# Expert tokens in one tile of 384 each and then in blocks of 128, in a fused attention, MLP and mixture-of-experts kernel

## The chip, the core and the metric

The kernel runs on one core of one Trainium2 chip. The metric is the device time of a run in microseconds (us). The engines are named as the profile names them: PE is TensorE (PEld its weight loads), DVE is VectorE, ACT is ScalarE, POOL is GpSimd, SP is the queue that issues most DMAs.

## The reference

```
N, D, E, F = 2304, 512, 8, 1024
x = attention(q, k, v)                  # 4 x 8 heads, 576 positions, window 128
x = (s * relu(x @ w_in)**2 + b) @ w_out # 512 -> 2048 -> 512
logits = x @ w_gate
noisy  = logits + log1p(exp(x @ w_noise)) * noise
top2, top2_w = the two largest of 8, softmax of the two
for e in range(8):
    for k in range(2):
        mask = top2[:, k] == e
        h = max(x[mask] @ w1[e], 0)
        out[mask] += top2_w[mask, k] * (h @ w2[e])
```

Each of the 2304 tokens goes to two of the eight experts, so the experts see 4608 token rows. With the inputs of the reference (a fixed seed) its own routing, worked out from its formulas, gives the experts 514, 463, 581, 704, 662, 654, 542 and 488 tokens.

## The kernel before, in words

All matrix products take a value as a rounded part and a rest (`..._hi` and `..._lo`) and make three matmuls of it (`three`, L1132 to L1134).

Stage one (T1 = 6 tiles of 384 tokens) interleaves the attention with the dense MLP; in each tile a loop over 16 chunks of the hidden size makes a slot of 12 matmuls over 384 columns (`first_product`) and 9 over 512 (`second_product`). The routing of the tile before is threaded through the slots: `turn_x2` transposes its output, `logits` (L1158) multiplies it with `w_route` so that the logits come out as 16 rows, DVE copies them (`copy_logits`, L788) and `turn_logits` (L1165) transposes them; `choose` and `assign` then find experts and places, and POOL scatters each token row (512 values and 4 words that go with it: two weights, its place, its number) to two rows of `rows_scratch` in DRAM. `rows_scratch` and `y_scratch` are partly filled with zeros by SP in the first tile's slots (L404, L407).

Stage two is the experts. A short table (DVE, `table`) holds how many tiles of TOK2 = 256 tokens an expert has, at least two; the last tile of an expert is moved back so that it ends with its last token, and tiles may so overlap. A loop runs over the tiles of an expert on each engine, with the engines held together by semaphores that count tiles. One tile `i`:

- SP: `load_rows(i + 1)` (L417) after the rows before are turned and after DVE has read the words that go with them (`meta_used`); in the first tile of an expert it also loads the next expert's eight weight chunks; after `r_ready` it writes the result to `y_scratch` (L436).
- PE: eight chunks `c`, `first_product` with 128 rows of weights as the stationary operand and the 256 tokens as the moving one (12 matmuls of 256 columns) and, two chunks later (`LAG`), `second_product` with the hidden values stationary and 512 weight columns moving (6 matmuls of 512 columns); `turn_rows(i + 1)` (L1257, eight transposes) stands two `second_product`s from the end.
- ACT: relu into `g_hi` (L679), the next expert's weights (L667), then the rounding of the turned rows (L661).
- DVE: the rest `g_lo` (L1024), `indices` and `whole_indices` (the index words, L983 to L1007), the rests of the weights (L1015) and of the rows (L959), and last the result `x2` (L1039), weight times product plus what was fetched.
- POOL: gathers the other expert's share of each token from `y_scratch` (L493) and scatters the result to the output (L501). A token's second expert adds the first one's result to its own.

The buffers are single: `rows`, `xm_hi`, `xm_lo` hold one tile, so the load of the next rows waits until the words that go with the rows of this one are read.

Of the kernel before, what the change touches and what calls it, by code (L numbers as in the profile page):

```python
# [9 lines left out]
ALU = mybir.AluOpType  # L10
# [3 lines left out]
P = 128  # L14
# [19 lines left out]
TOK2, BLK2 = 256, 2  # L34
NBLK = N // P
GMAX = N * 2 // TOK2 + 2 * E
# [65 lines left out]
def build(nc, a, out):  # L102
# [8 lines left out]
    with ctx:  # L111
# [12 lines left out]
        logits_t = sb("logits_t", [2 * E, TOK1], F32)  # L124
# [41 lines left out]
        out_to = sb("out_to", [P, BLK2], I32)  # L166
        first_row = sb("first_row", [P, E + 1], F32)
# [92 lines left out]
        lg_copied = sem("lg_copied")  # L260
        lg_turned = sem("lg_turned")
# [22 lines left out]
        tile_done = sem("tile_done")  # L284
# [5 lines left out]
        out_done = sem("out_done")  # L290

# [44 lines left out]
        def tile_at(eng, e, least_at):  # L336

            return eng.value_load(bounds[0:1, bass.ds(e, 1)], min_val=least_at, max_val=GMAX - 2 + least_at)

        def tiles_of(eng, pr, par):  # L340

            return tile_at(eng, pr * 2 + par, 0), tile_at(eng, pr * 2 + par + 1, 2)

        with nc.Block() as block:
            @block.sync
            def _(sp):
# [48 lines left out]
                for t in range(T1):  # L395
                    for c in range(C1 + LAG):
# [18 lines left out]
                def load_rows(i):  # L415
                    r = 0 if isinstance(i, int) else sp.value_load(starts[0:1, bass.ds(i, 1)], min_val=0, max_val=ROWS - TOK2)
                    sp.dma_start(rows[:], rows_dram[bass.ds(r, TOK2), :].rearrange("(b p) d -> p b d", p=P)  # L417
                                 ).then_inc(rows_in, 16)

                def tile(i, chunks=None):  # L420
                    if chunks is not None:
                        q0, ks = chunks
                        for k in ks[:C2 // 2]:
                            load_weights(sp, load_later(sp, q0 + k), k % STAGES)
                    sp.wait_ge(turned, i * BLK2 + BLK2)
# [4 lines left out]
                    if chunks is not None:  # L430
                        for k in ks[C2 // 2:]:
                            load_weights(sp, load_later(sp, q0 + k), k % STAGES)
# [15 lines left out]
                with sp.Fori(0, E // 2 - 1) as pr:  # L448
                    for par in range(2):
                        expert(pr, par, range(STAGES, STAGES + C2))  # L450
# [897 lines left out]
```

## Time and profile before

| | |
|---|---|
| time, median of three runs | 1155.73 us (1154.34 to 1157.4) |
| time of the profiled execution | 1154.33 us |
| its span, first to last instruction | 1152.5 us |
| mean granted TensorE clock | 0.973 |
| PE busy | 1076.9 us, 93% |
| DVE busy | 677.6 us, 59% |
| ACT busy | 476.9 us, 41% |
| POOL busy | 137.3 us, 12% |

The profile is one execution. A busy PE means only that matmuls were in flight, so the pace of the matmuls (start to start) is read from the timeline and from the chain of waits. The chain is followed back from the last instruction, at each step to what released it. The granted clock is given as a share of full speed: 1.00 is 2.4 GHz, 0.50 is 1.2 GHz, and what lies between is a mean over a stretch.

### The profile page before, as it was taken

How to read it: one execution, taken by the hardware profiler on the slowest of the kernel's cores; microseconds unless marked ns; L12 is line 12 of the kernel's file. 1: busy time of each engine (PE TensorE's matmuls, PEld its weight loads, DVE VectorE, ACT ScalarE, POOL GpSimd, SP SyncE). 2: the span in 40 equal slices, each digit the busy share in tenths (PEclk: the TensorE clock that was granted, in tenths of full speed). 3: DMA queues.
4: the chain of work that ended last, by engine and by line, in shares of the span. 5: the costliest groups of instructions: out<-in, count | busy, mean ns of one | idle time of the engine just before them, and what ended most of it. 6: DMA issues, size and time to landing. Idle time of an engine off the chain costs nothing.

```text
span 1152.5 us, 20528 instructions
## 1 busy us (share of the span) xinstructions
PE 1076.9 (93%) x6751; PEld 965.5 (84%) x6752; DVE 677.6 (59%) x2006; ACT 476.9 (41%) x1036; POOL 137.3 (12%) x135
## 2 busy tenths in 40 slices
PE   5699799999999999999974999999999999999995
PEld 4588698888888888888854999999999999999994
DVE  6777566866866776754756537463635537354342
ACT  6656465555555555534532314231413214132111
POOL 0000000100110020020012211212121212112121
PEclk9799999999999999999996999999999999999998
DMA  6559922342342242132353515161522516243232
GB/s 186 148 193 361 324 79 87 105 126 92 101 134 90 84 161 74 44 109 88 121 172 108 168 37 185 63 208 49 183 83 90 192 61 206 95 137 104 69 107 73
DMA packets 80238, 146.90 MB, mean 127 GB/s; under 512 B 12924, under 2 KB 13564, under 8 KB 80176
## 3 DMA queue, kind: packets, MB, share of 16 engines
q1 hardware_dynamic: 70256, 125.36, 33.9%
q0 software_dynamic: 9920, 20.78, 5.3%
q8 instruction: 30, 0.49, 0.2%
q14 instruction: 32, 0.26, 0.1%
HBM read 111.14 MB, written 46.77 MB: 137 GB/s over the span
## 4 chain that ended last, share of the span: by engine, by line
PE 81%; DVE 5%; ACT 5%; issue 4%; SPq 3%; DMA 1%; POOL 0%; POOLq 0%; DVEq 0%; ACTq 0%
PE bank L1132 24%; PE bank L1133 23%; PE bank L1134 23%; PE bank L1113 3%; PE bank L1257 2%; PE bank L1100 2%; PE bank L1158 1%; ACT x_sc L525 1%; PE bank L1079 1%; SPq L351 1%; PE bank L1080 1%; DVE x_sc L721 1%; ACT w_now_hi L579 1%; SPq L407 1%; ACT qk_hi L513 1%
## 5 line engine op out<-in xcount | busy, mean ns | idle before, releaser
L679 ACT ACTIVATE g_hi<-bank 128x256 fp32r<-128x256 f32 x176 | 67.7, 384 | 347.7 <-PE bank L1134 331.6
L1024 DVE SCALAR_TENSOR_TENSOR g_lo<-bank,g_hi 128x256 fp32r<-128x256 f32 x176 | 74.5, 423 | 183.3 <-ACT g_hi L679 183.2
L1132 PE MATMUL bank<-w_hi,g_hi 128*128 128x512 f32 x336 | 136.0, 405 | 0.0
L1133 PE MATMUL bank<-w_lo,g_hi 128*128 128x512 f32 x336 | 131.8, 392 | 0.0
L1134 PE MATMUL bank<-w_hi,g_lo 128*128 128x512 f32 x336 | 131.2, 391 | 0.0
L585 ACT ACTIVATE relu<-bank 128x384 f32<-128x384 f32 x96 | 47.1, 490 | 168.4 <-PE bank L1134 159.3
L1132 PE MATMUL bank<-xm_hi,w_hi 128*128 128x256 f32 x384 | 109.1, 284 | 1.5 <-DVE xm_lo L959 1.5
L1134 PE MATMUL bank<-xm_hi,w_lo 128*128 128x256 f32 x384 | 109.3, 285 | 0.0
L1133 PE MATMUL bank<-xm_lo,w_hi 128*128 128x256 f32 x384 | 109.3, 285 | 0.0
L468 POOL DMA_INDIRECT rows_scratch<-x,slot x36 | 38.4, 1067 | 533.0 <-DVE x L861 523.9
L776 DVE SCALAR_TENSOR_TENSOR relu<-relu,sb_scale 128x384 f32<-128x384 f32 x96 | 59.3, 618 | 65.8 <-ACT relu L585 64.6
L1134 PE MATMUL bank<-xm_hi,w_other_lo 128*128 128x256 f32 x320 | 90.6, 283 | 0.0
L1133 PE MATMUL bank<-xm_lo,w_other_hi 128*128 128x256 f32 x320 | 90.5, 283 | 0.0
L1132 PE MATMUL bank<-xm_hi,w_other_hi 128*128 128x256 f32 x320 | 90.2, 282 | 0.0
L1132 PEld LDWEIGHTS bank<-xm_hi,w_hi 128*128 128x128 f32 x384 | 74.2, 193 | 4.9 <-issue 1.9
L525 ACT ACTIVATE x_sc<-x_sc,least 128x256 f32<-128x256 f32 (+1 forms) x144 | 69.9, 488 | 19.0 <-DVE least L721 18.7
L1133 PEld LDWEIGHTS bank<-xm_lo,w_hi 128*128 128x128 f32 x384 | 74.2, 193 | 2.8
L493 POOL DMA_INDIRECT spare<-y_scratch,y_from x44 | 51.4, 1169 | 202.6 <-DVEq L1009 171.7
L1134 PEld LDWEIGHTS bank<-w_hi,g_lo 128*128 128x128 f32 x336 | 63.1, 188 | 14.2
L770 DVE TENSOR_TENSOR w_now_lo<-stage_a,w_now_hi 128x1024 fp32r<-128x1024 f32 x48 | 58.6, 1221 | 27.8 <-ACT w_now_hi L579 25.1
L1134 PEld LDWEIGHTS bank<-xm_hi,w_lo 128*128 128x128 f32 x384 | 74.1, 193 | 0.0
L721 DVE CUSTOM_DVE_ANT_0 x_sc<-bank,nbias 128x256 f32<-128x256 f32 (+1 forms) x144 | 52.9, 405 | 34.5 <-PE bank L1080 26.3
(177 smaller groups left out, 2774.8 us busy)
## 6 DMA issues: line engine op xcount, KB each, us to landing
stage_a<-in_w_first SPq DMA_DIRECT2D x92, 256.0 KB
stage_a<-in_w_second SPq DMA_DIRECT2D x92, 256.0 KB
y_scratch<-x SPq DMA_DIRECT2D x41, 512.0 KB, 7.2
qk_raw<-in_qk SPq DMA_DIRECT2D x144, 128.0 KB, 2.7
rows<-rows_scratch SPq DMA_DIRECT2D x23, 516.0 KB
stage_b<-in_w_first SPq DMA_DIRECT2D x28, 256.0 KB
stage_b<-in_w_second SPq DMA_DIRECT2D x28, 256.0 KB
v_sb<-in_vp SPq DMA_DIRECT2D x18, 256.0 KB, 2.9
```

The lines of the kernel that those rows point to most:

```text
L468: pool.indirect_dma_start(out=rows_dram, out_offset=bass.IndirectOffsetOnAxis(ap=slot[:, j, k:k + 1], axis=0), in_=x2[:, j, :], in_offset= ...
L493: pool.indirect_dma_start(out=fetched[:, j, :], out_offset=None, in_=y_dram, in_offset=bass.IndirectOffsetOnAxis(ap=y_from[:, j:j + 1], ax ...
L525: done = act.activation(x_sc[:, i % XS, s, 0:keys], x_sc[:, i % XS, s, 0:keys], ACT.Exp, scale=-1.0, bias=least[:, hp, s:s + 1], accum_out ...
L585: act.activation(relu[:, (t * C1 + c) % GR, :], h_bank[c % 2][:, 0:TOK1], ACT.Relu).then_inc(relu_ready, 1)
L679: act.activation(g_hi[:, c % GR, 0:TOK2], h_bank[c % 2][:, 0:TOK2], ACT.Relu).then_inc(gh2_ready, 1)
L721: done = dve.tensor_tensor_reduce(out=x_sc[:, i % XS, s, 0:keys], in0=s_of(i)[:, s * 256:s * 256 + keys], in1=nbias[:, 2 * hp + s, first:f ...
L770: dve.tensor_tensor(ring_a(1, p), stage(r % EARLY), ring_a(0, p).bitcast(F32), ALU.subtract).then_inc(w_ready, 1)
L776: dve.scalar_tensor_tensor(out=r, in0=r, scalar=sb_scale[:, 0:1], in1=r, op0=ALU.mult, op1=ALU.mult).then_inc(sq_ready, 1)
L1024: dve.scalar_tensor_tensor(out=g_lo[:, c % GR, 0:TOK2], in0=h_bank[c % 2][:, 0:TOK2], scalar=0.0, in1=g_hi[:, c % GR, 0:TOK2].bitcast(F32) ...
L1132: pe.matmul(psum, lh, rh, start=(first and n == 0), stop=False)
L1133: pe.matmul(psum, lh, rl, start=False, stop=False)
L1134: done = pe.matmul(psum, ll, rh, start=False, stop=(last and n == len(pairs) - 1))
```

## The change

Each expert now takes one tile of 384 tokens (`tile(e)`, TOK2 = 384), built as before but with three blocks of 128, and then blocks of 128 tokens (`single`), at least one. With the counts above that is 8 tiles and 2, 1, 2, 3, 3, 3, 2 and 1 blocks, 17 in all. The weights of the next expert are loaded and split in the tile.

In a block both products have 128 tokens as the stationary operand and 512 weight columns as the moving one: `block_first` makes the 1024 hidden values in two halves (12 matmuls each), with tokens down the partitions; relu goes to `hidden`, `turn_hidden` transposes a half (four transposes), ACT rounds it to `gb_hi` and DVE makes `gb_lo`; `block_second` makes eight chunks of three matmuls. `turn_block(i + 1)`, four transposes of the next block's rows, stands half way through the `block_second`s. The block has its own semaphores (`b_...`) and its own row buffer `rows_1`, also single. On DVE the increment of `b_meta_used`, for which SP waits before `load_block(i + 1)`, stands behind both halves of `gb_lo`. On POOL a block has one gather and one scatter.

In stage one the logits are made with the tokens stationary and `w_route` moving (16 columns), so they come out by tokens: `copy_logits` and `turn_logits` are gone, and `logits` moves from slot 3 to slot 5. `fetched` and the table's work space lie in `x2T`. The zero writes are 24 of 258 KB and 13 of 768 KB (before: 16 of 258 KB and 19 of 512 KB), and `y_scratch` is zeroed up to slot 14 in place of slot 11.

The core of the diff (left out: semaphores, POOL's part, the table's formulas, the parts of `tile` that only change names):

```diff
-TOK2, BLK2 = 256, 2
+TOK2, BLK2 = 384, 3
 NBLK = N // P
-GMAX = N * 2 // TOK2 + 2 * E
+GMAX = (2 * N - 2 * TOK2) // P + E
...
-        logits_t = sb("logits_t", [2 * E, TOK1], F32)
...
+        xb_hi = sb("xb_hi", [P, KD, P], F32R)
+        xb_lo = sb("xb_lo", [P, KD, P], F32R)
         rows = sb("rows", [P, BLK2, RW], F32)
-        spare = sb("spare", [P, 4 * G * E], F32)
+        rows_1 = sb("rows_1", [P, 1, RW], F32)
+        spare = x2T[:].rearrange("p k n -> p (k n)")
...
+        hidden = relu[:].rearrange("p r n -> p (r n)")[:, 0:F2]
+        gb_hi = g_hi[:].rearrange("p r n -> p (r n)")[:, 0:F2]
+        gb_lo = g_lo[:].rearrange("p r n -> p (r n)")[:, 0:F2]
...
+        b_out, b_rows, b_turned = bank[0], bank[2], bank[6:8]
...
-                            for r in range((c - 2) * 2 * TOK2, min((c - 1) * 2 * TOK2, YROWS), TOK2):
-                                sp.dma_start(y_dram[r:r + TOK2, :].rearrange("(p b) d -> p b d", b=2),
-                                             x2[:, 1:3, 0:DM]).then_inc(zero_out, 16)
+                            for r in range((c - 2) * TOK2, min((c - 1) * TOK2, YROWS), TOK2):
+                                sp.dma_start(y_dram[r:r + TOK2, :].rearrange("(p b) d -> p b d", b=BLK2),
+                                             x2[:, :, 0:DM]).then_inc(zero_out, 16)
...
+                def load_block(i):
+                    r = sp.value_load(starts[0:1, bass.ds(i, 1)], min_val=0, max_val=ROWS - P)
+                    sp.dma_start(rows_1[:], rows_dram[bass.ds(r, P), :].rearrange("(b p) d -> p b d", p=P)
+                                 ).then_inc(b_rows_in, 16)
...
+                def tile(e, later, ks):
+                    for k in ks[:C2 // 2]:
+                        load_weights(sp, load_later(sp, e * C2 + k), k % STAGES)
+                    if later:
+                        sp.wait_ge(turned, e * BLK2 + BLK2)
+                        sp.nop(nofuse=True)
+                        sp.wait_ge(meta_used, e + 1)
+                        sp.nop(nofuse=True)
+                        load_rows(e + 1)
+                    for k in ks[C2 // 2:]:
+                        load_weights(sp, load_later(sp, e * C2 + k), k % STAGES)
+                    sp.wait_ge(r_ready, e + 1)
                     sp.nop(nofuse=True)
-                    sp.wait_ge(meta_used, i + 1)
+                    r = sp.value_load(y_first[0:1, bass.ds(e, 1)], min_val=0, max_val=YROWS - TOK2)
+                    sp.dma_start(y_dram[bass.ds(r, TOK2), :].rearrange("(b p) d -> p b d", p=P),
+                                 x2[:, :, 0:DM]).then_inc(y_out, 16)
+
+                def single(i):
+                    sp.wait_ge(b_turned_x, i + 1)
                     sp.nop(nofuse=True)
-                    load_rows(i + 1)
-                    if chunks is not None:
-                        for k in ks[C2 // 2:]:
-                            load_weights(sp, load_later(sp, q0 + k), k % STAGES)
-                    sp.wait_ge(r_ready, i + 1)
+                    sp.wait_ge(b_meta_used, i + 1)
+                    sp.nop(nofuse=True)
+                    load_block(i + 1)
+                    sp.wait_ge(b_r_ready, i + 1)
                     sp.nop(nofuse=True)
                     r = sp.value_load(y_starts[0:1, bass.ds(i, 1)], min_val=0, max_val=YROWS - TOK2)
-                    sp.dma_start(y_dram[bass.ds(r, TOK2), :].rearrange("(b p) d -> p b d", p=P),
-                                 x2[:, 0:BLK2, 0:DM]).then_inc(y_out, 16)
-
-                def expert(pr, par, ks):
-                    lo, hi = tiles_of(sp, pr, par)
-                    tile(lo, ((pr * 2 + par) * C2, ks) if ks else None)
-                    with sp.Fori(lo + 1, hi) as i:
-                        tile(i)
+                    sp.dma_start(y_dram[bass.ds(r, P), :].rearrange("(b p) d -> p b d", p=P),
+                                 x2[:, 0:1, 0:DM]).then_inc(b_y_out, 16)
+
+                def expert(e, later, ks):
+                    tile(e, later, ks)
+                    with sp.Fori(first_of(sp, e), end_of(sp, e)) as i:
+                        single(i)
...
+                def single(i):
+                    for half in range(2):
+                        cols = slice(half * DM, (half + 1) * DM)
+                        act.wait_ge(b_h_ready, i * 2 + half + 1)
+                        act.activation(hidden[:, cols], h_bank[half][:], ACT.Relu).then_inc(b_relu_ready, 1)
+                        act.wait_ge(b_h_turned, i * 2 + half + 1)
+                        act.activation(gb_hi[:, cols], b_turned[half][:], ACT.Copy).then_inc(b_gh_ready, 1)
+                    round_block(i + 1)
+
+                def expert(e, par, more=True, later=True):
+                    lo = first_of(act, e)
+                    tile(e, lo, more, (1 - par) * C2, later)
+                    with act.Fori(lo, end_of(act, e)) as i:
+                        single(i)
...
+                def rest_of_block(i):
+                    dve.wait_ge(b_xh_ready, i + 1)
+                    dve.tensor_tensor(xb_lo[:], b_rows[:].rearrange("p (k n) -> p k n", k=KD),
+                                      xb_hi[:].bitcast(F32), ALU.subtract).then_inc(b_xl_ready, 1)
...
+                            dve.wait_ge(rows_in, e * 16 + 16)
+                            indices(meta, e, rows[:, :, DM:RW], BLK2, region[:, 0, bass.ds(e, 1)], y_from[:])
+                            dve.sem_inc(meta_ready, 1)
                         if c == 4:
-                            whole_indices(i)
-                        if q0 is not None:
-                            rest_of_later(q0, c, other + c)
-                    rest_of_rows(i + 1)
-                    dve.wait_ge(tile_done, i + 1)
-                    dve.wait_ge(fetched_in, i * (BLK2 * 16) + BLK2 * 16)
-                    dve.wait_ge(y_out, i * 16)
-                    dve.wait_ge(out_done, i * (BLK2 * 16))
+                            dve.wait_ge(out_done, e * (BLK2 * 16))
+                            dve.tensor_scalar(out_to[:], sought[:, 1, :], NOWHERE, None, ALU.add
+                                              ).then_inc(meta_used, 1)
...
+                def single(e, i):
+                    dve.wait_ge(b_rows_in, i * 16 + 16)
+                    indices(b_meta, i, rows_1[:, :, DM:RW], 1, start_f[:, bass.ds(i, 1)], y_from_1[:])
+                    dve.sem_inc(b_meta_ready, 1)
+                    for half in range(2):
+                        cols = slice(half * DM, (half + 1) * DM)
+                        dve.wait_ge(b_gh_ready, i * 2 + half + 1)
+                        dve.tensor_tensor(gb_lo[:, cols], b_turned[half][:], gb_hi[:, cols].bitcast(F32), ALU.subtract
+                                          ).then_inc(b_gl_ready, 1)
+                    dve.wait_ge(b_out_done, i * 16)
+                    dve.tensor_scalar(out_to_1[:], sought[:, 1, 0:1], NOWHERE, None, ALU.add).then_inc(b_meta_used, 1)
+                    rest_of_block(i + 1)
+                    dve.wait_ge(b_done, i + 1)
+                    dve.wait_ge(b_fetched_in, i * 16 + 16)
+                    dve.wait_ge(y_out, e * 16 + 16)
+                    dve.wait_ge(out_done, e * (BLK2 * 16) + BLK2 * 16)
+                    dve.wait_ge(b_y_out, i * 16)
+                    dve.scalar_tensor_tensor(out=x2[:, 0, 0:DM], in0=b_out[:], scalar=w_tile[:, 0:1],
+                                             in1=fetched[:, 0, :], op0=ALU.mult, op1=ALU.add).then_inc(b_r_ready, 1)
...
-                            done = pe.matmul(to[0:2 * E, j * P:(j + 1) * P], w_route[:, k, :],
-                                             x2T[:, k, j * P:(j + 1) * P], start=(k == 0), stop=(k == KD - 1))
+                            done = pe.matmul(to[:, j * 2 * E:(j + 1) * 2 * E], x2T[:, k, j * P:(j + 1) * P],
+                                             w_route[:, k, :], start=(k == 0), stop=(k == KD - 1))
...
+                def turn_block(i):
+                    pe.wait_ge(b_rows_in, i * 16 + 16)
+                    for k in range(KD):
+                        done = pe.transpose(b_rows[:, k * P:(k + 1) * P], rows_1[:, 0, k * P:(k + 1) * P], ident[:])
+                    done.then_inc(b_turned_x, 1)
...
+                def block_first(par, half, ks):
+                    w = (w_hi, w_lo) if par == 0 else w_other
+                    cs = slice(half * C2 // 2, (half + 1) * C2 // 2)
+                    for k in ks:
+                        done = three(h_bank[half][:], [
+                            (xb_hi[:, k, :], xb_lo[:, k, :], w[0][:, cs, k * P:(k + 1) * P],
+                             w[1][:, cs, k * P:(k + 1) * P])], k == 0, k == KD - 1)
+                    return done
+
+                def turn_hidden(i, half):
+                    pe.wait_ge(b_relu_ready, i * 2 + half + 1)
+                    for k in range(KD):
+                        at_ = half * DM + k * P
+                        done = pe.transpose(b_turned[half][:, k * P:(k + 1) * P], hidden[:, at_:at_ + P], ident[:])
+                    done.then_inc(b_h_turned, 1)
+
+                def block_second(par, cs):
+                    w = (w_hi, w_lo) if par == 0 else w_other
+                    for c in cs:
+                        done = three(b_out[:], [
+                            (gb_hi[:, c * P:(c + 1) * P], gb_lo[:, c * P:(c + 1) * P],
+                             w[0][:, c, DM:CW], w[1][:, c, DM:CW])], c == 0, c == C2 - 1)
+                    return done
+
+                def single(e, par, i, later):
+                    pe.wait_ge(b_xl_ready, i + 1)
+                    block_first(par, 0, range(KD)).then_inc(b_h_ready, 1)
+                    block_first(par, 1, range(KD // 2))
+                    if later:
+                        pe.wait_ge(xl2_ready, e + 2)
+                    turn_hidden(i, 0)
+                    block_first(par, 1, range(KD // 2, KD)).then_inc(b_h_ready, 1)
+                    pe.wait_ge(r_ready, e + 1)
+                    pe.wait_ge(b_r_ready, i)
+                    pe.wait_ge(b_gl_ready, i * 2 + 1)
+                    block_second(par, range(C2 // 4))
+                    turn_hidden(i, 1)
+                    block_second(par, range(C2 // 4, C2 // 2))
+                    turn_block(i + 1)
+                    pe.wait_ge(b_gl_ready, i * 2 + 2)
+                    block_second(par, range(C2 // 2, C2)).then_inc(b_done, 1)
+
+                def expert(e, par, later=True):
+                    lo = first_of(pe, e)
+                    tile(e, par, lo, later)
+                    with pe.Fori(lo, end_of(pe, e)) as i:
+                        single(e, par, i, later)
```

## Rows read from the trace of the kernel before

**Rows 1.** Stretches: us, each engine's busy us (instructions), clock, DMA share, GB/s.
```profile
623.14:1140.05 516.91, 516.89 (x3344) 470.83 (x3344) 254.71 (x692) 144.66 (x276) 94.04 (x86) 1.00 0.36 118
...
160.00:590.00 430.00, 423.71 (x2608) 376.82 (x2607) 292.30 (x890) 231.03 (x521) 32.34 (x30) 1.00 0.33 104
...
84.00:130.00 46.00, 44.07 (x269) 39.36 (x268) 34.10 (x87) 29.27 (x65) 0.00 (x0) 1.00 1.04 354
```

**Rows 2.** Chain of waits in stage two: start us, us, engine and line.
```profile
632.04 0.23 PE bank L1132
...
634.86 0.23 PE bank L1132
...
668.16 0.87 PE bank L1257 x8
...
691.57 0.87 PE bank L1257 x8
```

**Rows 3.** Groups by form: operation, count, busy us, mean ns, idle time before.
```profile
L1132 PE MATMUL bank<-xm_hi,w_hi 128*128 128x256 f32 x384 | 109.1, 284 | 1.5 <-DVE xm_lo L959 1.5
...
L1132 PE MATMUL bank<-xm_hi,w_other_hi 128*128 128x256 f32 x320 | 90.2, 282 | 0.0
...
L1039 DVE SCALAR_TENSOR_TENSOR x<-bank,w_tile,spare 128x512 f32<-128x512 f32 x44 | 31.0, 746 | 31.2 <-PE bank L1134 31.2
...
L959 DVE TENSOR_TENSOR xm_lo<-bank,xm_hi 128x512 fp32r<-128x512 f32 x46 | 29.7, 685 | 28.6 <-ACT xm_hi L661 28.6
L661 ACT ACTIVATE xm_hi<-bank 128x512 fp32r<-128x512 f32 x46 | 25.1, 596 | 43.0 <-PE bank L1257 43.0
...
L1007 DVE TENSOR_SCALAR out_to<-sought 128x2 int32<-128x2 f32 x22 | 3.5, 159 | 0.0
```

**Rows 4.** Timeline of PE in stage one: start us, us, the matmul.
```profile
562.02 0.33 PE L1132 MATMUL bank<-x_hi,w_hi 128*128 128x384 f32 x1
...
564.13 0.39 PE L1132 MATMUL bank<-w_hi,g_hi 128*128 128x512 f32 x1
```

**Rows 5.** Timelines of ACT, DVE and SP around a transpose and a load.
```profile
692.04 1.09 ACT L661 ACTIVATE xm_hi<-bank 128x512 fp32r<-128x512 f32 x2 [1.36 <-PE bank L1257]
...
655.17 0.23 DVE L997 TENSOR_TENSOR sought<-sought,role 128x2 f32<-128x2 f32 x2
...
656.33 0.40 SPq L417 DMA_DIRECT2D rows<-rows_scratch  x1
```

**Rows 6.** The page, part 6: DMA, count, KB each, median us to landing.
```profile
y_scratch<-x SPq DMA_DIRECT2D x41, 512.0 KB, 7.2
...
v_sb<-in_vp SPq DMA_DIRECT2D x18, 256.0 KB, 2.9
```

**Rows 7.** Chain of waits, the first load of rows.
```profile
615.86 3.71 DMA rows<-rows_scratch
```

**Rows 8.** Stretches around idle gaps of PE; columns as in rows 1.
```profile
41.80:44.20 2.40, 0.17 (x2) 0.00 (x0) 1.47 (x4) 1.85 (x5) 0.29 (x1) 1.00 0.57 162
...
46.40:50.90 4.50, 0.35 (x2) 0.00 (x0) 3.15 (x10) 2.52 (x6) 0.00 (x0) 0.50 0.56 160
...
134.50:139.39 4.89, 0.24 (x2) 0.03 (x1) 3.55 (x11) 3.61 (x9) 0.00 (x0) 0.91 1.06 392
139.39:143.10 3.71, 3.71 (x33) 3.38 (x33) 2.35 (x5) 1.37 (x2) 0.00 (x0) 0.50 0.59 168
...
145.00:148.00 3.00, 3.00 (x18) 2.83 (x17) 0.60 (x4) 1.09 (x3) 0.00 (x0) 0.95 0.02 5
...
66.70:70.10 3.40, 3.40 (x15) 3.30 (x14) 3.06 (x9) 2.62 (x7) 0.00 (x0) 0.51 0.67 222
```

**Rows 9.** Chain of waits between the two stages, the last logits.
```profile
595.89 2.81 PE bank L1158 x24
...
598.72 0.56 DVE logits_t L788
...
599.32 0.37 PE bank L1165 x3
```

More of the change, by code:

```diff
@@ L483, in _, with tile @@
                     scatter(t)
-                pool.wait_ge(table_ready, 1)
-                n_tiles = pool.value_load(bounds[0:1, E:E + 1], min_val=1, max_val=GMAX)
-                with pool.Fori(0, n_tiles) as i:
-                    pool.wait_ge(meta_ready, i + 1)
-                    pool.wait_ge(y_out, i * 16)
+                def tile(e):
+                    pool.wait_ge(meta_ready, e + 1)
+                    pool.wait_ge(y_out, e * 16)
+                    pool.wait_ge(b_y_out, first_of(pool, e) * 16)
                     pool.nop(nofuse=True)
@@ L667, in round_later, with tile @@
                     act.activation(ring(0, place), stage(k % STAGES), ACT.Copy).then_inc(w_hi_done, 1)
-                def tile(i, q0=None, other=0, after=None):
-                    hi = None
+                def tile(e, lo, more, other, later):
                     for c in range(C2):
-                        if after is not None and c == C2 - 2:
-                            hi = tile_at(act, after, 2)
-                        act.wait_ge(h2_ready, i * C2 + c + 1)
+                        act.wait_ge(h2_ready, e * C2 + c + 1)
@@ L683, in tile @@
-                    round_rows(i + 1)
-                    return hi
-                def expert(pr, par, lo, more=True):
-                    hi = tile(lo, (pr * 2 + par) * C2 if more else None, (1 - par) * C2, pr * 2 + par + 1)
-                    with act.Fori(lo + 1, hi) as i:
-                        tile(i)
-                    return hi
+                            act.wait_ge(b_done, lo)
+                        act.activation(g_hi[:, c % GR, :], h_bank[c % 2][:, 0:TOK2], ACT.Relu).then_inc(gh2_ready, 1)
@@ new lines, in tile @@
+                        if more:
+                            round_later(e * C2, c, other + c)
+                    if later:
+                        round_rows(e + 1)
+                def single(i):
[6 more added lines that the diff above has]
+                    round_block(i + 1)
@@ L998, in indices @@
                     link(done)
[L999 to L1007 removed]
+                    dve.memset(fetched[:, 0:nb], 0.0)
@@ L1016, in rest_of_later, with tile @@
                                       ).then_inc(w_ready, 1)
-                def tile(i, q0=None, other=0, after=None):
-                    hi = None
+                def tile(e, lo, more, other, later):
                     for c in range(C2):
-                        if after is not None and c == C2 - 2:
-                            hi = tile_at(dve, after, 2)
-                        dve.wait_ge(gh2_ready, i * C2 + c + 1)
-                        dve.scalar_tensor_tensor(out=g_lo[:, c % GR, 0:TOK2], in0=h_bank[c % 2][:, 0:TOK2],
-                                                 scalar=0.0, in1=g_hi[:, c % GR, 0:TOK2].bitcast(F32),
+                        dve.wait_ge(gh2_ready, e * C2 + c + 1)
+                        dve.scalar_tensor_tensor(out=g_lo[:, c % GR, :], in0=h_bank[c % 2][:, 0:TOK2],
+                                                 scalar=0.0, in1=g_hi[:, c % GR, :].bitcast(F32),
@@ L1038, in tile @@
+                        if more:
+                            rest_of_later(e * C2, c, other + c)
+                    if later:
+                        rest_of_rows(e + 1)
+                    dve.wait_ge(chunk2_used, e * C2 + C2)
+                    dve.wait_ge(fetched_in, e * (BLK2 * 16) + BLK2 * 16)
+                    dve.wait_ge(y_out, e * 16)
+                    dve.wait_ge(b_y_out, lo * 16)
+                    dve.wait_ge(b_out_done, lo * 16)
                     for j in range(BLK2):
@@ L1041, in tile, with single @@
                     done.then_inc(r_ready, 1)
-                    return hi
-                def expert(pr, par, lo, more=True):
-                    hi = tile(lo, (pr * 2 + par) * C2 if more else None, (1 - par) * C2, pr * 2 + par + 1)
-                    with dve.Fori(lo + 1, hi) as i:
-                        tile(i)
-                    return hi
+                def single(e, i):
+                    dve.wait_ge(b_rows_in, i * 16 + 16)
[16 more added lines that the diff above has]
+                                             in1=fetched[:, 0, :], op0=ALU.mult, op1=ALU.add).then_inc(b_r_ready, 1)
@@ L1050, in _, with expert @@
+                def expert(e, par, more=True, later=True):
+                    lo = first_of(dve, e)
+                    tile(e, lo, more, (1 - par) * C2, later)
+                    with dve.Fori(lo, end_of(dve, e)) as i:
+                        single(e, i)
                 rest_of_rows(0)
+                rest_of_block(0)
                 with dve.Fori(0, E // 2 - 1) as pr:
-                    lo = tile_at(dve, pr * 2, 0)
                     for par in range(2):
-                        lo = expert(pr, par, lo)
```

251 lines of the change are left out of this document (126 added, 125 removed).

## The prediction

> **What bounds the kernel now.** I read first the busy time of each engine by stretch. The reader is to see that PE is the bound of both stages: 516.89 of 516.91 us in stage two, with the clock at 1.00 throughout, and 423.71 of 430 us in five sixths of stage one [rows 1]. No other engine is near that. Then I read the chain of waits in stage two, which is PE from end to end. The reader is to see two periods: 2.82 us from chunk to chunk (632.04 to 634.86) and 23.41 us from tile to tile (668.16 to 691.57), with the eight transposes of the next rows at 0.87 us in it, 0.109 each [rows 2]. A chunk is 12 matmuls of 256 columns and 6 of 512; at 0.23 for one of 512 [rows 2] that leaves 0.12 for one of 256. The groups by form give the tiles: 384 and 320 matmuls of one kind, 32 to a tile, are 12 and 10 tiles [rows 3], as the routed counts say (3, 2, 3, 3, 3, 3, 3, 2). So stage two is worth what PE's work in it is worth, as long as nothing stops PE. Last I looked for places where PE did stop, since the change gives it new waits; these are in the stretches around gaps [rows 8].
>
> **PE's work in stage two.** Before: 22 tiles of 256 are 5632 token slots. After: 8 x 384 + 17 x 128 = 5248. A slot of a 384 tile is 12 matmuls of 384 columns, which took 2.11 us in stage one (562.02 to 564.13) [rows 4], and 9 of 512 at 0.232 (between the 0.23 and 0.24 at which they run), 2.09; eight slots are 33.6. Eight tiles with seven times 12 transposes at 0.109 are 278.0. A block is 48 matmuls of 512 columns, 11.14, and 12 transposes, 1.31, together 12.45; 17 are 211.6. With 1.6 for the half clock at the start, as now, that is 491.2 against 516.9: minus 25.7. Without the 120 more transposes (13 us) it would be minus 39.
>
> **The wait that a block adds.** In `single` PE goes: half 0 (12 matmuls), two more of half 1's four steps, `turn_hidden(0)`, the rest of half 1, two chunks of `block_second`, `turn_hidden(1)`, two chunks, `turn_block(i + 1)`, four chunks. `turn_block(i + 1)` waits for `rows_1`; SP issues that load only after `b_meta_used`, and this increment stands on DVE behind both halves of `gb_lo`. So the load starts late, and I count from the start of `turn_hidden(1)`: 0.47 until ACT starts (691.57 to 692.04) [rows 2, 5]; the rounding 0.60 and the rest 0.69 [rows 3], with 0.06 between; the index operation 0.16 [rows 3]; 0.93 from the end of such a DVE operation (655.40) to SP's issue (656.33), in which SP reads the row number [rows 5]; the landing of 258 KB; 0.14 to PE. A load of 256 KB lands in 2.9 [rows 6], the load of two blocks of rows (516 KB) in 3.71 [rows 7]; I take 2.95, as the size is nearly that of the first. Sum 6.0 us. In that time PE has `turn_hidden(1)`, 0.44, and 6 matmuls, 1.40. PE then stands for 4.2 us, in each of the 17 blocks: plus 71.1. Bounds: 0.8 more each with the other landing, plus 14; nothing in the order of DVE's or SP's instructions lets it be less than about 3. Queued behind PE's wait are 12 matmuls, the next block or tile, and so all of ACT's and DVE's work.
>
> On the fixed part of that landing, the Trainium skill (DMA: Bandwidth & Descriptors, Anatomy of one DMA) has about 2.0 us for any DMA of POOL's path plus the bytes at 436 GB/s; by that, as an estimate, 258 KB take 2.6 us and the sum would be 5 us less. The load here goes by SP's queue, and the row of 2.9 decides.
>
> In an expert's first block a write of 768 KB to `y_scratch` comes just ahead of the load, on the same queue; writes of 512 KB took 7.2 [rows 6]. Issued 3.4 us after the tile's end (three result operations at 0.75 [rows 3], 0.93 of SP) it would still be landing when the load is issued at 10.5 (7.44 of PE's work in the block, then 3.05 of the chain above). I take 0.6 more for each of eight, plus 5 (0 to 10). The same write also delays the gather of the first block to some 16 us; the block ends at 16.7 and its result is needed 6 us later: nothing.
>
> The other waits of a block, worked out with the same durations: relu of half 0 is ready 0.6 us before PE wants it; `gb_lo` of half 0 ends as PE wants it (5.99 against 6.04); DVE's result operation and indices are over by then; `turn_block` to the next block's rests takes 1.8 us under 2.8 us of matmuls. Nothing, at most 0.2 a block. In a tile DVE has 33.6 us for the work it did in 23, and the next expert's weights land earlier against their use: nothing.
>
> **The clock.** An idle gap of 4.2 us has two like it in this trace. In the stretch of 46.40 to 50.90 PE was busy for 0.35 us and the clock at 0.50 all through; in that of 134.50 to 139.39 it was busy for 0.24, idle for 4.65, and the clock fell some 0.9 us before the end (0.91 over 4.89 us). A shorter one, 2.2 us idle in 41.80 to 44.20, kept 1.00 [rows 8]. After the fall PE ran at 0.50 from 139.39 until about 145.3, 5.9 us; another cold stretch lasted 3.4 us (66.70 to 70.10) [rows 8]. At half clock half the stretch is lost: 2.95 or 1.7, mean 2.3. As the fall came only just inside the gap of 4.65, I let seven in ten of the 17 gaps end cold: 17 x 0.7 x 2.3 = 27.6. Bounds: 0, and 17 x 3.2 = 54.7, if all that follows the gap in a block (four transposes and 12 matmuls) runs at half.
>
> **Stage one and the joints.** The logits keep 24 matmuls a tile (2.81 us [rows 9]), with 16 columns moving in place of 128 but 128 columns of weights in place of 16. From above they cost as the transposes do, which load as many (0.109, 2.6 us); from below I have only that the moving part shrinks, and let it go to 1.6. I take 2.1. With the three small transposes that is 1.0 a tile, minus 5 for five tiles (1 to 8), in a stage where PE is the bound. On the way to stage two the copy (0.56), the transposes (0.37) [rows 9] and 0.7 of logits fall away; a third block of rows brings 0.8 of landing (the 3.71 against 2.9 above) and 0.75 of rounding and rest: minus 0.1. At the end one of two result operations falls away (0.75 [rows 3]): minus 0.7; the one scatter less is left at nil.
>
> The zero writes grow from 13.9 to 16.2 MB. To slot 9 they come at the old rate, in a stretch where the DMA engines are full (share 1.04, 354 GB/s [rows 1]) and PE nonetheless busy; 2.3 MB more, 6.5 us at that rate, fall into slots 11 to 14, where PE's gap before 139.39 stands. I take plus 2 (minus 3 to plus 6.5).
>
> **Sum.** 1152.5 - 25.7 + 71.1 + 5 + 27.6 - 5 - 0.1 - 0.7 + 2 = 1226.7 of span; 1.8 lie around it (1154.33 - 1152.5), so 1228.5 for such an execution, whose time before was 1.4 below the median of the runs. I predict 1228.
>
> **The rivals.**
> - The clock holds in the gaps, as in that of 2.2 us: minus 27.6, 1201. For it: the fall at 4.65 came late in the gap. Against it: both gaps over 4 us ended at half.
> - The clock falls in each gap and the rest of the block is cold: plus 27, 1255. The Trainium skill (TensorE: Matmul & The Clock Gate, HAM oscillation) has this for a loop that waits for a DMA in each pass: it falls to the half rate in each. By that rule it would be 1255; the two long gaps here agree with it.
> - The load takes longer, beside gather, scatter and write of the same blocks: 1.5 us more in 17 blocks is 25, 1254. For it: writes of twice the size took 7.2 [rows 6].
> - Other side, faster: the rows of the next block are there when PE comes for them, so that neither stall, contention nor clock cost anything: 1228.5 - 71.1 - 5 - 27.6 = 1125. It decides at 1.7 us a block: 29.5 us are gained without stalls, over 17. For it is only that DMAs land in 3 us while a block lasts 12.5; against it is that the load's issue is tied to the last third of the block.
> - The change doesn't do what it says, as the counts of blocks differ: each block more or less is 18 us with its stall. The 12 and 10 tiles speak for the counts.
>
> **How the numbers follow.** Forecast, with its own range of 1210 to 1246: 0.45. Clock falls each time: 0.2. Clock holds: 0.15. Longer load: 0.1. Hidden load: 0.05. The rest, 0.05, lies outside on both sides. The range of 1192 to 1258 takes in the first four. A measurement can tell about 0.3% (3.5 us) from no change: faster 0.05, same 0.02, slower 0.93.
>
> **What would show it.** In the changed profile: the group of `turn_block`'s transposes with 17 or 18 waits on the DMA of `rows_1`, some 4 us each; before it SP waiting for DVE; a granted clock under 1.00 in the stretches of blocks and 1.00 in the tiles; a tile in 34.9 us and a block in 16.7 warm, 19 cold; more bytes written at 130 to 145 us. I am wrong if the load is issued before `turn_hidden(1)`, if it lands in under 1 us, or if another wait in a block (the second rest, the fetched rows) is longer than this one.

## The result and the profile after

The changed kernel takes 1234.17 us, median of 6 runs (1228.59 to 1235.94), beside 1155.45 us (1152.99 to 1157.58) of the kernel before: a ratio of 1.068, 95% interval 1.066 to 1.070. The forecast was 1228, range 1192 to 1258. The profiled execution has a span of 1226.8 us; the sum of the forecast gave 1226.7. That execution, at 1228.59 us, is the fastest of the six. Measured once more, beside the later experiments, the changed kernel was at 1.065 (1.063 to 1.068).

First the stretches of the changed kernel: stage two, the tail, and then one block (677.32 to 695.57) cut at its wait. Columns are us, busy us of PE, PEld, DVE, ACT and POOL with instructions, granted clock, DMA share, GB/s.

```profile
623.45:1216.97 593.52, 528.77 (x2448) 449.08 (x2448) 240.78 (x658) 146.39 (x226) 83.91 (x81) 0.93 0.30 98
1216.97:1226.80 9.83, 0.17 (x1) 0.00 (x0) 0.75 (x1) 0.00 (x0) 1.01 (x1) 0.64 0.14 53
...
677.32:686.82 9.50, 9.39 (x45) 7.28 (x43) 4.06 (x19) 2.39 (x4) 2.05 (x2) 1.00 0.08 29
686.99:690.74 3.75, 0.00 (x1) 0.01 (x1) 0.02 (x1) 0.00 (x0) 0.00 (x0) 0.99 0.28 70
690.74:694.17 3.43, 3.43 (x11) 2.90 (x11) 0.69 (x1) 0.60 (x1) 0.00 (x0) 0.51 0.02 5
694.17:695.57 1.40, 1.40 (x8) 1.13 (x6) 0.00 (x0) 0.00 (x0) 0.00 (x0) 1.00 0.00 0
```

Stage two lasts 593.5 us where it lasted 516.9 [rows 1], 76.6 more, which is the whole loss (the span grew by 74.3, as the tail is shorter); it begins at 623.45 where it began at 623.14. PE is no longer busy throughout (528.77 of 593.52), and the clock is at 0.93. In the block all engines are idle for 3.75 us while 16 DMA engines are 28% busy, and after it PE runs at half clock for 3.4 us.

The waits of PE in stage two (what waited, for whom, us in total, times, longest):

```profile
PE bank L1327 <- DMA rows<-rows_scratch: 62.9, 17, 3.9
```

L1327 is the transposes of `turn_block`. Before, PE waited 16.3 us in all for such a load, once, ahead of the stage; now 17 times more, once in each block. The only other wait in the list for this stage is one of 0.8 us; waits as short as 0.1 us are not in it. The chain of waits through one of the 17 (start us, us, what):

```profile
685.15 0.45 PE bank L1362 x4
...
685.63 0.61 ACT g_hi L751
...
686.26 0.05 DVE g_lo L1108
686.31 0.55 issue
686.87 0.16 DVE out_to L1111
...
687.10 0.05 SPq L442
...
687.92 2.77 DMA rows<-rows_scratch
...
690.74 1.12 PE bank L1327 x4
```

This is the path that was counted out beforehand: the turn of the second half (L1362), the rounding, the rest (the "issue" of 0.55 is the body of that operation), the index operation, SP's reading of the row number (L442), the load and the transposes. From the turn's start at 684.99 to 690.74 it is 5.75 us, where the forecast had 6.0. The landing took 2.77 for 2.95 and the step from DVE to SP's issue 0.90 for 0.93; the start of the rounding came 0.64 us behind the turn's start for 0.47.

### The profile page after: what moved, and what is told of

Read it like the earlier page. It is cut to its first block, busy times and chain, and to the rows that moved or that the text cites. A ratio compares the mean times of both kernels' runs of the same rounds, so it can differ in the third digit from the quotient of the medians.

```text
span 1226.8 us, 18393 instructions
## 1 busy us (share of the span) xinstructions
PE 1088.4 (89%) x5845; PEld 948.0 (77%) x5846; DVE 661.0 (54%) x1967; ACT 480.1 (39%) x988; POOL 126.5 (10%) x130
## 4 chain that ended last, share of the span: by engine, by line
PE 76%; issue 6%; DMA 5%; DVE 5%; ACT 5%; SPq 1%; POOL 0%; ACTq 0%; DVEq 0%; POOLq 0%
PE bank L1208 22%; PE bank L1209 21%; PE bank L1210 21%; DMA rows<-rows_scratch 4%; PE bank L1189 3%; PE bank L1176 2%; PE bank L1327 1%; PE bank L1234 1%; PE bank L1155 1%; ACT x_sc L583 1%; PE bank L1362 1%; PE bank L1320 1%; PE bank L1156 1%; DMA stage_a<-in_w_second 1%; ACT g_hi L751 1%
## 5 line engine op out<-in xcount | busy, mean ns | idle before, releaser
L739 ACT ACTIVATE g_hi<-bank 128x384 fp32r<-128x384 f32 x64 | 31.5, 492 | 170.9 <-PE bank L1210 168.1
L1076 DVE SCALAR_TENSOR_TENSOR g_lo<-bank,g_hi 128x384 fp32r<-128x384 f32 x64 | 35.6, 556 | 82.9 <-ACT g_hi L739 76.0
L1327 PE MATMUL bank<-ident,rows 128*128 128x128 f32 x72 | 19.1, 418 | 62.9 <-DMA rows<-rows_scratch 62.9
L1208 PEld LDWEIGHTS bank<-w_hi,g_hi 128*128 128x128 f32 x312 | 62.9, 201 | 15.3 <-issue 4.6
L1208 PE MATMUL bank<-w_other_hi,g_hi 128*128 128x512 f32 x160 | 71.2, 445 | 0.9
L1209 PEld LDWEIGHTS bank<-w_lo,g_hi 128*128 128x128 f32 x312 | 62.7, 201 | 10.1
L1208 PE MATMUL bank<-x_hi,w_hi 128*128 128x384 f32 x192 | 67.3, 351 | 1.8 <-DVE x_lo L809 1.7
L749 ACT ACTIVATE relu<-bank 128x512 f32<-128x512 f32 x34 | 20.3, 598 | 123.4 <-PE bank L1210 123.4
L1209 PE MATMUL bank<-w_other_lo,g_hi 128*128 128x512 f32 x160 | 68.6, 429 | 0.0
L1210 PE MATMUL bank<-w_other_hi,g_lo 128*128 128x512 f32 x160 | 68.1, 426 | 0.0
L1208 PE MATMUL bank<-x_hi,w_now_hi 128*128 128x384 f32 x192 | 66.8, 348 | 0.1
L1327 PEld LDWEIGHTS bank<-ident,rows 128*128 128x128 f32 x72 | 12.5, 210 | 70.2 <-DMA rows<-rows_scratch 70.2
```

The lines of the kernel that those rows point to most:

```text
L1076: dve.scalar_tensor_tensor(out=g_lo[:, c % GR, :], in0=h_bank[c % 2][:, 0:TOK2], scalar=0.0, in1=g_hi[:, c % GR, :].bitcast(F32), op0=ALU. ...
L1208: pe.matmul(psum, lh, rh, start=(first and n == 0), stop=False)
L1209: pe.matmul(psum, lh, rl, start=False, stop=False)
L1210: done = pe.matmul(psum, ll, rh, start=False, stop=(last and n == len(pairs) - 1))
L1327: done = pe.transpose(b_rows[:, k * P:(k + 1) * P], rows_1[:, 0, k * P:(k + 1) * P], ident[:])
```

## The experiments

The kernels were measured in two groups, each on one chip together with the kernel before. It gave 1151.58 us beside the early leave, the fills of 16 and 8 matmuls and the logits alone, and 1153.84 beside the others; ratios are to it, and times of different groups are compared by ratio.

### The leave given early

The increment for which SP waits moves up; the one left behind goes to a new semaphore for which nothing waits.

```diff
                     dve.sem_inc(b_meta_ready, 1)
+                    dve.sem_inc(b_meta_used, 1)
...
-   dve.tensor_scalar(out_to_1[:], sought[:, 1, 0:1], NOWHERE, None, ALU.add).then_inc(b_meta_used, 1)
+   dve.tensor_scalar(out_to_1[:], sought[:, 1, 0:1], NOWHERE, None, ALU.add).then_inc(b_out_to, 1)
```

> The kernel after the change, with one edit: in a block DVE gives SP leave to load the next block's rows right behind the index words, in place of behind both rests of the hidden values. Theory (the late leave makes the wait, 3.9 us in each of 17 blocks, and the clock that falls in that gap costs 2.1 more in each): both go, 66 + 36 us, and the time is 1132 us (1128 to 1142), the clock 1.00 through the blocks. Rival (a block of 128 tokens has a second wait just behind the first, the relu, turn and rounding chain or the gather of what is added): the wait moves, PE still stands over 2 us a block and the time stays over 1165.

Measured: 1132.6 us (1129.66 to 1134.97), ratio 0.983 (0.981 to 0.986). Its stage two, and PE's waits in it:

```profile
624.59:1122.28 497.69, 493.55 (x2448) 424.11 (x2448) 240.77 (x658) 146.46 (x227) 83.89 (x81) 1.00 0.36 117
```

```profile
PE bank L1329 <- DMA rows<-rows_scratch: 2.0, 4, 1.0
PE bank L1210 <- DVE xm_lo L1022: 0.6, 1, 0.6
PE bank L1210 <- DVE g_lo L1110: 0.2, 1, 0.2
```

Moving one semaphore increment takes 95.8 us out of stage two (593.5 to 497.7). The wait for the rows falls from 62.9 us to 2.0 and no wait takes its place that is longer than it was (the short one for the first rest, 0.28 us a block, was there before and is still), so the rival, a second wait close behind, falls. The changed kernel with this edit beats both kernels, the one before by 1.7%.

### The gap filled with matmuls

```diff
                     block_second(par, range(C2 // 4, C2 // 2))
+                    w_any = w_hi if par == 0 else w_other[0]
+                    for _ in range(16):
+                        pe.matmul(bank[1][:], gb_hi[:, 0:P], w_any[:, 0, DM:CW], start=True, stop=True)
                     turn_block(i + 1)
```

> The kernel after the change, with 16 more matmuls of 512 columns in each block ahead of the transposes that wait for the rows, into a bank that nobody reads (results are unchanged). They take 3.7 us, the length of the idle gap, so the load is as late as before but PE isn't idle. Theory (66 us of the loss are the wait and 36 the half clock after it): only the clock's part goes, 1234 - 36 = 1198 us, clock 1.00. Rival (the clock costs nothing of its own, as the chain of the next block has slack for it): 1234, unchanged.

Measured: 1193.84 us (1188.77 to 1194.69), ratio 1.037 (1.035 to 1.039). Stage two:

```profile
620.22:1177.16 556.94, 554.74 (x2720) 472.75 (x2720) 240.67 (x658) 146.51 (x226) 84.09 (x81) 1.00 0.32 105
```

PE has 272 more matmuls to do and the kernel is faster than the changed one, at a ratio of 1.037 for 1.065, which is 32 us. The load is as late as before: a block takes as long up to `turn_block`. All that differs is that PE isn't idle, and the clock stays at 1.00. In the profiles stage two is 593.5 - 556.9 = 36.6 us shorter. The transposes began 0.1 us sooner in each block, 1.7 us of it, so the clock by itself costs 35 us. That fits what the changed profile has: 16 stretches from `turn_block` to the end of a block took 33.4 us more than the 3.25 that each takes here, and the last one, cut short by the end of the stage, 1.6 more. From 556.9 to 497.7, 59.2 us, is the wait by itself.

With 8 of these matmuls:

> As the one with 16 added matmuls, but with 8 (1.9 us), which leave PE idle for about 2.0 us in each block. Theory (a short gap leaves the clock alone, as one of 2.2 us did before the change): 1198 us, as with 16. Rival (any gap of 2 us in each block is enough): half clock after the gaps and 1215 to 1234.

Measured: 1192.53 us (two executions, 1191.11 and 1193.95), ratio 1.036 (1.033 to 1.038). Stage two, and PE's wait in it:

```profile
623.30:1182.05 558.75, 526.50 (x2584) 449.11 (x2584) 240.74 (x658) 146.54 (x227) 84.10 (x81) 1.00 0.32 105
```

```profile
PE bank L1327 <- DMA rows<-rows_scratch: 30.3, 17, 1.9
```

Here PE stands for 1.8 us in each of 17 blocks (1.7 to 1.9) and the clock is at 1.00 all the same: these gaps cost only themselves. With 4:

> With 4 added matmuls of 512 columns (0.93 us) ahead of the wait in each block of the changed kernel: an idle gap of about 2.8 us, between the 1.9 that left the clock at 1.00 and the 3.7 that always ended at 0.50. If the clock falls in each: as after the change, 1230. If it holds: 1193, as with 8 and 16. In between: it falls in a share of the gaps. I expect a share of a third, 1205.

Measured: 1208.94 us (two executions, 1207.49 and 1210.39), ratio 1.048 (1.045 to 1.051). PE's wait, stage two, a gap with the stretch behind it that kept the clock, and one that lost it:

```profile
PE bank L1327 <- DMA rows<-rows_scratch: 46.3, 17, 2.8
```

```profile
622.26:1195.90 573.64, 525.41 (x2516) 447.06 (x2516) 240.56 (x658) 146.42 (x226) 83.89 (x81) 0.97 0.31 102
...
783.00:789.37 6.37, 3.56 (x18) 2.61 (x17) 0.75 (x2) 0.60 (x1) 1.27 (x2) 1.00 0.25 64
789.37:792.60 3.23, 3.23 (x16) 2.75 (x17) 0.69 (x1) 0.60 (x1) 0.00 (x0) 1.00 0.00 0
...
888.80:891.40 2.60, 0.00 (x0) 0.00 (x0) 0.00 (x0) 0.00 (x0) 0.00 (x0) 0.86 0.40 102
891.45:897.50 6.05, 6.05 (x17) 4.89 (x18) 0.69 (x1) 0.60 (x1) 0.00 (x0) 0.50 0.00 0
```

The stretch behind the gap, four transposes and 12 matmuls, takes 3.25 us at full clock. Of the 16 blocks that have it whole, 7 took 3.25 to 3.27 and 9 took 4.5 to 6.0. So gaps of the same length, 2.6 to 2.8 us, fall on either side. The mean share was nearer a half than the third that was expected; the time was within 4 us of it.

### The leave between the two rests

```diff
                                           ).then_inc(b_gl_ready, 1)
+                        if half == 0:
+                            dve.sem_inc(b_meta_used, 1)
```

> The kernel after the change, with the leave for the next rows between the two rests of the hidden values (behind the first), in place of behind both and the index operation. Theory (only the place of the leave counts): the leave comes 6.0 us into a block, the rows 3.7 us later at 9.7 (0.90 to SP's issue, 2.82 to PE), PE wants them at 9.3 to 9.5: 0.2 to 0.5 us of wait in place of 3.9, no fall of the clock, 1134 to 1142 us. Rival (the load is slow in this place of the block whenever it is issued, beside the gather): over 1150.

Measured: 1132.13 us (1128.48 to 1135.89), ratio 0.982 (0.980 to 0.985). Stage two, and PE's wait for the rows:

```profile
620.96:1116.85 495.89, 491.81 (x2448) 422.32 (x2448) 240.74 (x658) 146.48 (x227) 83.91 (x81) 1.00 0.36 118
```

```profile
PE bank L1330 <- DMA rows<-rows_scratch: 1.8, 3, 1.2
```

It is as good as the early leave. From start to start the rows cost 3.5 us in all, 0.2 a block, the low end of what was expected. Away from an expert's first block the load is issued 6.3 us into a block and lands in 2.6 to 3.1 us, against 2.6 to 2.8 when it is issued 10.6 us in, so the rival falls.

That both places of the leave do equally well has a second reason. All that is left of the wait stands in the experts' first blocks, and there the early leave brings the load no sooner than this one. Issues of SP in the first block of the first expert, with the early leave and with this one:

```profile
664.61 0.43 SPq L461 DMA_DIRECT2D y_scratch<-x  x1
668.15 0.35 SPq L444 DMA_DIRECT2D rows<-rows_scratch  x1
...
659.25 0.43 SPq L461 DMA_DIRECT2D y_scratch<-x  x1
662.79 0.35 SPq L444 DMA_DIRECT2D rows<-rows_scratch  x1
```

In all eight experts of both kernels the load is issued 3.5 to 3.8 us behind the tile's write, some 7 us into the block. With the early leave DVE's last index operation ended at 666.19, so that the issue came 1.96 us behind it in place of 0.90: something else than the leave held it. What SP does in that time no run here settles.

### The first half turned one step sooner

```diff
-                    block_first(par, 1, range(KD // 2))
+                    block_first(par, 1, range(1))
...
-                    block_first(par, 1, range(KD // 2, KD)).then_inc(b_h_ready, 1)
+                    block_first(par, 1, range(1, KD)).then_inc(b_h_ready, 1)
```

> The kernel with the early leave, and the first half's hidden values turned after one step of the second half in place of two. PE waited 0.28 us in each block for the first rest, the second wait of a block. Theory: it goes and the turn waits under 0.1 for the relu instead, minus 4 us against the early leave alone, 1129. Rival (relu is late by the whole step): no gain, 1133 to 1137.

Measured, on top of the early leave: 1129.56 us (1129.01 to 1134.28), ratio 0.981 (0.978 to 0.983). Stage two:

```profile
623.49:1117.95 494.46, 491.92 (x2448) 421.78 (x2448) 240.52 (x658) 146.48 (x226) 84.02 (x81) 1.00 0.36 118
```

Stage two is 3.2 us shorter in the profile than with the early leave alone, where the theory had 4; but it is 1.4 us shorter than with the leave between the rests, which should equal the early leave. What the edit itself does is seen in a block without a wait for rows: 12.53 us for 12.67, 2.4 in 17. The wait for the first rest fell from 0.28 to 0.02 a block, and the turn came 0.17 late for the relu, where the theory had under 0.1. In the times the two intervals overlap (0.978 to 0.983 and 0.981 to 0.986), so that it is the faster of the two isn't shown by them.

### The logits alone, in the kernel before

```diff
-                            done = pe.matmul(to[0:2 * E, j * P:(j + 1) * P], w_route[:, k, :],
-                                             x2T[:, k, j * P:(j + 1) * P], start=(k == 0), stop=(k == KD - 1))
+                            done = pe.matmul(to[:, j * 2 * E:(j + 1) * 2 * E], x2T[:, k, j * P:(j + 1) * P],
+                                             w_route[:, k, :], start=(k == 0), stop=(k == KD - 1))
```

The copy, the small transposes and their waits are taken out too.

> The kernel before, with the routing logits alone made as after the change: tokens stationary, 16 columns moving, no copy and no second transpose. The forecast had 1.0 us a tile and 1.6 at the joint, 1149 to 1150 us. What the trace of the changed kernel shows (24 matmuls in 2.75 us, 2.79 before) speaks for the rival: the weight loads of 128 columns set the pace and nothing is saved but the copy and the small transposes, about 1 us at the joint and 0.3 in each other tile, 1153 us.

Measured: 1151.24 us (12 executions), ratio 0.9996 (0.9985 to 1.0008). The logits' group in the kernel before and in this one (form, count, busy us, mean ns, idle before):

```profile
L1158 PE MATMUL bank<-x2T,w_route 128*16 128x128 f32 x144 | 16.8, 273 | 0.8 <-ACT x2T L604 0.8
```

```profile
L1148 PE MATMUL bank<-w_route,x2T 128*128 128x16 f32 x144 | 16.8, 261 | 0.8 <-ACT x2T L601 0.8
```

16 columns in place of 128 take the same busy time, 16.8 us for 144 records (each `pe.matmul` of these f32 operands stands in the profile as two). No difference can be measured; a gain of up to 1.7 us is not excluded. The expected 1153 was 2 us under a kernel before of 1155; that much is excluded, if barely.

### The changed kernel again

> The changed kernel once more, so that it stands beside the others on one chip: a ratio of 1.068 to the kernel before.

Measured: 1229.77 us (1226.23 to 1231.27), ratio 1.065 (1.063 to 1.068). Its profile has the same waits, and all 16 stretches behind them took 4.7 to 6.0 us as before:

```profile
PE bank L1327 <- DMA rows<-rows_scratch: 61.8, 17, 3.8
```

## Why the prediction held, point by point

**PE's work.** Forecast 491.2 us for stage two without waits. With the early leave stage two took 497.7 us, of which 3.4 are for the rows from start to start and 4.8 for the first rest (below): 489.5. The kernel with the leave between the rests gives 487.6 in the same way. The step holds: 516.9 less 488 to 490 is 27 to 29 us, forecast 25.7. No run takes it apart further; the forecast's account is 384 token slots fewer, less the added transposes.

**The wait of a block.** Right in place, order and size. Forecast 4.2 us from start to start; the changed profile has 62.9 us in 17 waits, 3.7 each behind the end of the last matmul, 3.9 from start to start. That is 66 against 71: the landing took 2.8 in place of 3.1 with the step to PE. The rival of a longer load falls with it: none of the 17 took over 2.9 us. That there are 17 waits also bears out the count of blocks.

**Contention with the tile's write.** Forecast 5 us, measured none: the eight waits in an expert's first block are 3.6 to 3.9 us long, the others 3.5 to 3.8. The step that failed is the duration of the write. The 7.2 us for 512 KB [rows 6] are the median of the 19 zero writes of stage one alone, made in a stretch with full DMA engines [rows 1]; the trace has no landing for the 22 writes of tiles. In the changed kernel the first tile's write of 768 KB is issued at 661.74 and the load of the next block's rows at 668.79. The stretches between (columns as above) and two groups of its DMAs (size, median us to landing):

```profile
662.50:664.80 2.30, 2.19 (x12) 1.56 (x11) 1.33 (x5) 1.04 (x2) 1.69 (x3) 1.00 0.92 340
664.80:668.79 3.99, 3.09 (x16) 2.21 (x14) 0.75 (x2) 0.75 (x2) 1.99 (x2) 1.00 0.04 2
...
rows<-rows_scratch SPq DMA_DIRECT2D x18, 258.0 KB, 2.7
y_scratch<-x SPq DMA_DIRECT2D x17, 256.0 KB, 2.1
```

The write moves at 340 GB/s and is over some 3 us after its issue, 4 us before the load.

**A wait that was set at nothing.** PE stood some 0.28 us in each block before `block_second`, for the first rest: 683.03 to 683.54 from one matmul to the next where 0.23 is the pace. That is 5 us in all, where the forecast had "at most 0.2 a block". It had the rest ready 1.81 us after the turn's start (5.99 less the 4.18 of the matmuls before it) and PE wanting it 0.05 later. In this block PE could go on 2.11 us after the turn's start (681.43 to 683.54): the rounding started 0.17 later than counted, and the step from DVE's end to PE, 0.15, was left out. Turning one step sooner gained 2.4 us.

**The clock.** The term was right in kind and too small: 27.6 forecast, 35 by the filled gaps. It failed in its form. It had seven in ten gaps fall and 2.3 us lost in each; in the changed profile all 16 stretches that can be read fell (4.6 to 6.0 us where 3.2 is the warm time), with 2.1 lost in each. Of the two long gaps that it leaned on, that of 46.40 to 50.90 [rows 8] was no case of a gap that makes the clock fall. Just before it, in the kernel before, PE was busy for four transposes, and the clock fell then already (columns as above):

```profile
45.95:46.75 0.80, 0.80 (x4) 0.41 (x4) 0.79 (x2) 0.80 (x4) 0.00 (x0) 0.73 0.80 166
```

The rival in which the clock holds is refuted. That in which it falls each time had the right count and the wrong price, 3.2 each: in the block above PE was back at full clock after 3.4 us (694.17), before the block was over, and only the longest of the 16 stretches, 6.0 us, was cold to its end (granted clock 0.50). The price went with the clock's fall: 1.4 to 1.6 us in the seven blocks in which the gap itself still had 0.94 or more, 2.3 to 2.8 in the nine in which it had 0.76 to 0.88. By the Trainium skill (TensorE: Matmul & The Clock Gate, HAM oscillation) a loop that stands for a DMA in each pass, in its example for some 3 to 5 us, falls to half rate in each. The changed profile agrees with it, 16 of 16 with waits of 3.5 to 3.9 us. The runs with shorter gaps add that a wait in each pass isn't enough, as 17 waits of 1.8 us left the clock at 1.00.

**Stage one and the joints.** Forecast minus 5 for the logits, plus 2 for the zero writes, minus 0.1 for the joint; the start of stage two moved by plus 0.3. That 0.3 is loose: among the eight profiles with this stage one the start lies between 620.22 and 624.59, and there is one profile of the kernel before (623.14). The step that failed is the logits' pace. They load 128 columns of weights for 16 that move and ran at 0.115 us (24 in 2.75), above the 0.109 of the transposes that I had taken as the end from above; the value of 0.09 was between that row and no row at all. The experiment on the kernel before gives 0.3 us less (between 1.7 less and 0.9 more) for the tiles and the joint together, where the forecast had 6.6 less. The zero writes weren't tried alone, so their cost stays open: PE's two gaps near 130 and 140 us are still there, at 2.7 and 3.2 us for 1.8 and 4.65.

**The tail.** 9.7 us from the end of PE's last matmul (0.17 us into the tail's stretch above) to the end of the span, 12.5 before: minus 2.8 where the forecast had minus 0.7. The result operation less gives 1.0. The scatter less, which was left at nil, gives 1.3: before, the second was issued that much behind the first. The last 0.5 is open.

So the total was met by terms that missed in both directions: wait and contention 10 us too much, the clock 7 and the first rest 5 too little, stage one and the joint 3 too little, work and tail 2 each too much. Added up as measured (-28 + 66 + 5 + 35 + 0.3 - 2.8) they give 1228 of span for the 1226.8 of the profile. The kind and the order of the large terms were foreseen; that the sum met the span to 0.1 us is luck.

**Slips in the working.** By its own words (a profiled execution 1.4 below the median) the sum of 1228.5 is a median of 1230, not 1228; measured was 1234. A landing of 2.6 us in place of 2.95 takes 6 us off the sum over 17 blocks, not 5. In the time at which a first block's load is issued, 10.5, the 0.14 from landing to PE is counted, which comes later; measured was 10.6.

**The other side.** The rival that the rows are there in time had 1125 and its point of decision at 1.7 us a block. With the early leave and the sooner turn the kernel came to 1129.6. Its condition, though, was not met by the change as made: in DVE's order the leave stood behind the second rest and the index operation, and ahead of the second rest was early enough.

## What to carry to other kernels

When a loop body is cut into shorter ones, each wait in it is paid more often, and a load that was issued early in a long body may be issued late in a short one: count from the instruction that gives the leave to the one that needs the data, and compare that with the other work between them. Give a buffer free behind its last reader, and not behind whatever comes next on that reader's engine; here that one line was worth 96 us in stage two, more than three times what the smaller work gained, and 35 of them were the clock that fell in the gaps. Take a DMA's duration from transfers of the same size in the same stretch, not from a median over all.

## What the runs showed of the hardware

- Idle gaps of PE between dense matmuls, one in each block: of 1.8 us, none of 17 ended in half clock; of 2.7 us, 9 of 16; of 3.7 us, 16 of 16 in each of two profiles. The fills that shortened the gaps also lengthened PE's work between them, so the two weren't varied apart. With gaps of 3.7 us a fall cost 1.4 to 2.8 us of the work behind it, 2.1 in the mean.
- 272 matmuls that nobody needs, put into idle gaps, made the changed kernel faster by 32 us, from a ratio of 1.065 to 1.037.
- A write of 768 KB to DRAM, alone on the DMA engines, moved at 340 GB/s and was over some 3 us after its issue; the writes of 512 KB in the crowded start of the kernel before took 5.1 to 12.3.
- A matmul of f32 operands stands in the profile as two records. With 128 stationary and 16 moving columns it ran at the same pace as with 16 stationary and 128 moving: 0.115 and 0.116 us a record.
- SP needed 0.90 us from the end of a DVE operation to the issue of a load whose address it reads from memory, nearly a third of the landing.
